# Early expert scores of gathered rows alone, the skip score on VectorE, and values products in the half step of a later unit's scores

## The reference

```python
# 1. attention, B=4, H=8, S=576, D=64; heads 0-3 a local window of 32, heads 4-7 strided by 32
scores = np.where(masks[None], scale * np.matmul(q, k.transpose(0, 1, 3, 2)), -1e9)
attn = softmax(scores)                       # written out with max, exp and sum + 1e-9
x = np.matmul(attn, v)                       # -> (2304, 512)
# 2. dense layer, d_ff = 2048
h = x @ w_in
g = np.where(h >= 1, h, np.where(h <= -1, 0.0, (h + 1) ** 2 / 4))
x = g @ w_out
# 3. experts, E = 8, F = 1024
do_compute = x @ w_skip > 0                  # all other rows are passed on unchanged
xc = x[do_compute]
logits = xc @ w_gate
e_idx = np.argmax(logits, axis=1)            # one expert for each row
gate_w = softmax(logits)[row, e_idx]
out[do_compute] = xc + gate_w * (np.maximum(xc @ w1[e_idx], 0.0) @ w2[e_idx])
```

## Time and profile before

| what | value |
|---|---|
| median of 3 runs | 529.65 us (528.9 to 530.3) |
| the profiled execution's own time | 529.79 us |
| its span, first to last instruction | 527.9 us |
| PE, PEld (weight loads beside PE) | 97%, 83% of the span busy |
| DVE, ACT, POOL | 48%, 39%, 40% |
| granted TensorE clock, mean | 0.983 |

### The profile page before, as it was taken

The page is one execution under the profiler, slowest core; times in us unless marked ns, Lnnn a source line. Parts: engine busy times, 40 slices in busy tenths (PEclk is TensorE's granted clock), DMA queues, the critical chain, the costliest instruction groups (busy, mean ns, idle before and its releaser), DMA issues.

```text
span 527.9 us, 9196 instructions
## 1 busy us (share of the span) xinstructions
PE 512.3 (97%) x3546; PEld 439.2 (83%) x3546; DVE 251.3 (48%) x580; ACT 207.2 (39%) x461; POOL 211.5 (40%) x242
## 2 busy tenths in 40 slices
PE   5899998999999999999999999999999999999996
PEld 3687887889888888888888888888988988887895
DVE  5947657733226435646534646552322483222222
ACT  4956554553332324343433354433232223323122
POOL 0659787662222324544633444542221323221221
PEclk9769999999999999999999999999999999999999
DMA  8992201003001104201210420000300071840001
GB/s 250 343 382 98 70 28 52 31 2 119 1 1 52 64 24 165 76 3 34 91 45 1 166 76 32 2 1 22 115 6 1 0 259 62 299 161 1 2 0 63
DMA packets 19010, 42.22 MB, mean 80 GB/s; under 512 B 2084, under 2 KB 3952, under 8 KB 18964
## 3 DMA queue, kind: packets, MB, share of 16 engines
q1 hardware_dynamic: 18836, 41.59, 22.8%
q0 software_dynamic: 128, 0.02, 0.0%
HBM read 33.06 MB, written 8.78 MB: 79 GB/s over the span
## 4 chain that ended last, share of the span: by engine, by line
PE 88%; DVE 7%; ACT 2%; issue 1%; POOL 1%; DMA 1%; SPq 0%; DVEq 0%; ACTq 0%
PE bank L1004 37%; PE bank L1020 36%; PE bank L865 4%; PE bank L829 4%; PE bank L846 3%; PE bank L875 1%; DVE row_sum L1165 1%; PE bank L886 1%; DVE bank L1148 1%; DVE row_max L1153 1%; DMA qk<-in_qk_dram 1%; DVE prob L1155 1%; PE bank L951 1%; PE bank L932 1%; DVE prob_first L1139 1%
## 5 line engine op out<-in xcount | busy, mean ns | idle before, releaser
L1748 POOL TENSOR_TENSOR g_lo<-act_f,g_hi 128x384 fp32r<-128x384 f32 x96 | 97.1, 1012 | 202.2 <-ACT g_hi L1634 201.9
L1625 ACT ACTIVATE act_f<-act_f,half_col 128x384 f32<-128x384 f32 x96 | 59.2, 616 | 207.4 <-DVE act_f L1367 207.3
L1367 DVE TENSOR_SCALAR act_f<-bank 128x384 f32<-128x384 f32 x96 | 53.2, 554 | 159.7 <-PE bank L1004 155.9
L1004 PE MATMUL bank<-x_hi,win_hi 128*128 128x384 f32 x384 | 90.1, 354 | 0.6 <-DVE act_f L1370 0.6
L1020 PE MATMUL bank<-wout_hi,g_hi 128*128 128x512 f32 x285 | 86.2, 411 | 0.0
L1004 PE MATMUL bank<-x_hi,win_lo 128*128 128x384 f32 x384 | 84.4, 338 | 0.0
L1004 PE MATMUL bank<-x_lo,win_hi 128*128 128x384 f32 x384 | 83.8, 336 | 0.0
L1634 ACT CAST g_hi<-act_f 128x384 fp32r<-128x384 f32 x96 | 49.2, 512 | 84.8 <-DVE act_f L1370 83.9
L1020 PE MATMUL bank<-wout_lo,g_hi 128*128 128x512 f32 x285 | 81.1, 393 | 0.0
L1020 PE MATMUL bank<-wout_hi,g_lo 128*128 128x512 f32 x285 | 80.9, 392 | 0.0
L1004 PEld LDWEIGHTS bank<-x_hi,win_hi 128*128 128x128 f32 x384 | 65.8, 190 | 8.4 <-issue 2.8
(11 more groups left out here) (134 smaller groups left out, 469.2 us busy)
## 6 DMA issues: line engine op xcount, KB each, us to landing
w_early<-in_w_dram SPq DMA_DIRECT2D x4, 2048.0 KB, 8.7
qk<-in_qk_dram SPq DMA_DIRECT2D x12, 592.0 KB, 4.0
out_dram<-y_rows SPq DMA_DIRECT2D x18, 256.0 KB, 2.6
win_raw<-in_w_in_dram SPq DMA_DIRECT2D x16, 256.0 KB, 9.1
wout_raw<-in_w_out_dram SPq DMA_DIRECT2D x16, 256.0 KB, 9.4
y_dram<-y_rows SPq DMA_DIRECT2D x15, 256.0 KB, 2.8
v<-in_v_dram SPq DMA_DIRECT2D x6, 384.0 KB
v<-in_v_dram SPq DMA_DIRECT2D x6, 288.0 KB
```

The source lines that it names most:

```text
L1004: mm = pe.matmul(h_ps[s % 2][:, 0:CH], w[:, f, P * k:P * (k + 1)], x[:, k, cols], start=(at == 0), stop=(at == len(order) - 1))
L1367: dve.tensor_scalar(tile, h_ps[s % 2][:, 0:CH], -1.0, 1.0, ALU.max, ALU.min).then_inc(clip_ready, 1)
L1625: act.activation(tile, tile, ACT.Square, bias=half_col[:, 0:1], scale=0.5).then_inc(square_ready, 1)
L1748: pool.tensor_tensor(g_lo[:, s % RING, :], act_f[:, s % 2, :], g_hi[:, s % RING, :].bitcast(F32), ALU.subtract).then_inc(g_lo_ready, 1)
```

## The change

1. The score jobs `Y`, `Z`, `A` leave the trunk. The skip score of each 128 rows is made on DVE instead (`row_skip`: one 128x512 multiply-and-sum of `y_rows` and `w_skip`, both in SBUF, and its accumulator read), at places 6, 10 and 14 (4, 5, 6 in `c` = 4). The expert scores of all rows are made only in the branch behind the trunk, which now first loads the rows back.
2. The early experts choose rows by the skip score alone (at most 32 rows), from place 7 of `c` = 4 on; the rows are gathered once, turned, and only they are multiplied with `w_gate` (`gate`, 16 calls of 8 columns). Their experts are ranked, the two first experts that are present are loaded, and both tiles work on the same 32 rows; a row is scattered from the tile of its own expert.
3. `w_skip` is loaded at the start of `c` = 1 instead of in `c` = 5.
4. In `c` = 2 and 3 every `V` moves one place back; `S` and `P` stay. In `c` = 1 the second of the two units starts at place 24 instead of 22, and `P` and `V` of both come one place sooner after their `S`.

```diff
     if c == 1:
         for i in range(EARLY, PER_BATCH):
-            unit_at(N_PRO + REST + i, 18 + 4 * (i - EARLY), 5, 7)
+            unit_at(N_PRO + REST + i, 18 + 6 * (i - EARLY), 4, 6)
     if c in (2, 3):
         for i in range(PER_BATCH):
-            unit_at(N_PRO + REST + PER_BATCH * (c - 1) + i, 1 + 3 * i, 4, 5)
+            unit_at(N_PRO + REST + PER_BATCH * (c - 1) + i, 1 + 3 * i, 4, 6)
+    if c > 0:
+        for t, at in enumerate((4, 5, 6) if c == EARLY_CHUNKS else (6, 10, 14)):
+            got[at].append(("skip", CT * (c - 1) + t))
     if c == EARLY_CHUNKS:
-        for i in range(5):
-            got[19 + i].append(("rank", i))
-        got[21].append(("count", 0))
-        got[25].append(("weights", 0))
-        for i in range(2):
-            got[24 + i].append(("choose", i))
-            got[26 + i].append(("info", i))
-            got[27 + i].append(("ids", i))
-            got[28 + i].append(("gather", i))
+        for at, kind in ((7, "flag"), (9, "count"), (11, "slot"), (13, "choose"), (15, "info"), (16, "ids"),
+                         (17, "gather"), (20, "turn"), (22, "gate"), (23, "rank"), (25, "present"), (26, "experts"),
+                         (27, "weights")):
+            got[at].append((kind, 0))
     if c == EARLY_CHUNKS + 1:
-        got[4].append(("skip", 0))
         got[20].append(("left", 0))
...
         for i in range(2):
-            got[i].append(("turn", i))
...
-    if c > 0:
-        for at, job in zip((6, 8, 10, 12, 13, 15, 17), score_jobs(c - 1)):
-            got[at].append(job)
...
-PLACES_AFTER = [score_jobs(CHUNKS - 1)]
+SCORE_ORDER = [CHUNKS - 1] + list(range(CHUNKS - 1))
+PLACES_AFTER = [score_jobs(c) for c in SCORE_ORDER]
...
             for c in range(CHUNKS):
+                if c == 1:
+                    wait_full(sp, "V", N_PRO - 1)
+                    sp.dma_start(w_skip_sb[:, :], w_skip[:, :]).then_inc(w_skip_loaded, 16)
...
+            def early_gates():
+
+                take_bank(pe, "gate", 0)
+                wait_free(pe, "turn", 0)
+                for k in range(KT):
+                    for g in range(4):
+                        mm = pe.matmul(bank_of("gate", 0)[ES * g:ES * (g + 1), 0:E], e_rows_t[:, ES * k:ES * (k + 1)],
+                                       w_score[:, k, 0:E], start=(k == 0), stop=(k == KT - 1))
+                mm.then_inc(full_sem("gate", 0), 1)
...
+            def row_skip(q):
+
+                c, t = q // CT, q % CT
+                if q == 0:
+                    dve.wait_ge(w_skip_loaded, 16)
+                wait_rows(dve, c, t)
+                dve.tensor_tensor_reduce(out=skip_terms[:, :], in0=y_rows[:, t, :], in1=w_skip_sb[:, :], scale=1.0,
+                                         scalar=0.0, op0=ALU.mult, op1=ALU.add, accum_out=score[:, q, E:E + 1])\
+                   .then_inc(row_skips, 1)
+                dve.wait_ge(row_skips, q + 1)
...
                 for t in (0, 2):
                     if c > 0:
                         dve.wait_ge(y_stored[t], 32 * c)
-                        wait_full(dve, "Y", CT * (c - 1) + t)
+                        dve.wait_ge(row_skips, CT * c)
                     dve.tensor_copy(y_rows[:, t, :], y_ps[t][:, :]).then_inc(y_dve, 1)
...
+            def gather_early():
                 pool.wait_ge(e_placed, 4)
...
+                for t in range(CT):
+                    pool.wait_ge(y_stored[t], 32 * EARLY_CHUNKS)
+                pool.wait_ge(e_info_steps, 6)
+                pool.indirect_dma_start(out=e_rows[:, :], out_offset=None, in_=y_quarters[0:4 * P * ET, :],
+                                        in_offset=bass.IndirectOffsetOnAxis(ap=e_row_ids[:, 0:1], axis=0),
+                                        bounds_check=last_quarter, oob_is_err=False).then_inc(e_gathered, 16)
```

More of the change, by code:

```diff
@@ L171, in places_of_chunk @@
             got[8 + 11 * i].append(("second", i))
-    if c > 0:
-        for at, job in zip((6, 8, 10, 12, 13, 15, 17), score_jobs(c - 1)):
-            got[at].append(job)
     return got
 PLACES = [places_of_chunk(c) for c in range(CHUNKS)]
-PLACES_AFTER = [score_jobs(CHUNKS - 1)]
+SCORE_ORDER = [CHUNKS - 1] + list(range(CHUNKS - 1))
+PLACES_AFTER = [score_jobs(c) for c in SCORE_ORDER]
 def bank_table():
     n_banks = {"S": 2, "P": 2, "V": 1, "Y": 1, "Z": 1, "A": 1,
-               "count": 1, "info": 1, "turn": 1, "first": 1, "back": 1, "second": 1, "total": 1}
+               "count": 1, "info": 1, "turn": 1, "gate": 1, "present": 1, "first": 1, "back": 1, "second": 1,
+               "total": 1}
     used = [0] * 8
@@ L765, in _ @@
                             early_weights(n)
-                        if kind == "skip":
-                            sp.wait_ge(h_full, FT * (CHUNKS - 1))
-                            wait_full(sp, "info", 1)
-                            sp.dma_start(w_skip_sb[:, :], w_skip[:, :]).then_inc(w_skip_loaded, 16)
                     if c > 0 and at == 2 * LAG - 1:
@@ new lines, in early_gates, with early_present @@
+            def early_gates():
[6 more added lines that the diff above has]
+                mm.then_inc(full_sem("gate", 0), 1)
+            def early_present():
+                take_bank(pe, "present", 0)
+                pe.wait_ge(e_ranked, 2)
+                pe.matmul(bank_of("present", 0)[:, 0:E], et("ones"), e_onehot[:, :], start=True, stop=True)\
+                  .then_inc(full_sem("present", 0), 1)
@@ L961, in do_jobs @@
                     if kind == "info":
-                        early_info(n)
+                        early_info()
                     if kind == "turn":
-                        turn_early_rows(n)
+                        turn_early_rows()
+                    if kind == "gate":
+                        early_gates()
+                    if kind == "present":
+                        early_present()
                     if kind == "first":
@@ L1182, in keep_scores @@
                 tiles = score_tiles(n)
[L1183 removed]
                 rows = bank_of("A", n)[:, 0:SC * len(tiles)].rearrange("p (t e) -> p t e", e=SC)
[L1185 removed]
+                dve.tensor_copy(score[:, tiles[0]:tiles[-1] + 1, 0:E], rows[:, :, 0:E])\
                    .then_inc(free_sem("A", n), 1)
@@ L1255, in early_choose, with early_flags, early_slots @@
-            def early_choose(i):
+            def early_flags():
+                dve.wait_ge(row_skips, ET)
+                dve.wait_ge(e_table_loaded, 32)
+                early_link(dve.tensor_scalar(e_flags[:, :], score[:, 0:ET, E], 0.0, None, ALU.is_gt))
+            def early_slots():
+                counts = bank_of("count", 0)
+                wait_full(dve, "count", 0)
+                early_link(dve.tensor_tensor_scan(e_running[:, :], et("ones")[:, 0:ET], counts[:, 0:ET], 0.0,
+                                                  ALU.mult, ALU.add))
+                early_link(dve.tensor_scalar(e_over[:, :], e_running[:, ET - 1:ET], float(ES), None, ALU.is_gt))
+                early_link(dve.tensor_tensor(e_slot[:, :], e_running[:, :], counts[:, ET:2 * ET], ALU.subtract))
+                dve.sem_inc(free_sem("count", 0), 1)
+                early_link(dve.tensor_scalar(e_skipped[:, :], e_flags[:, :], 0.0, FAR, ALU.is_equal, ALU.mult))
+                early_link(dve.tensor_tensor(e_slot[:, :], e_slot[:, :], e_skipped[:, :], ALU.add))
@@ L1326, in do_jobs @@
                         count_left()
-                    if kind == "rank":
-                        early_rank(n)
-                    if kind == "choose":
-                        early_choose(n)
-                    if kind == "ids":
-                        early_ids(n)
+                    if kind == "skip":
+                        row_skip(n)
+                    if kind == "flag":
+                        early_flags()
+                    if kind == "slot":
+                        early_slots()
+                    if kind == "choose":
+                        early_choose()
+                    if kind == "ids":
+                        early_row_ids()
+                    if kind == "rank":
+                        early_rank()
+                    if kind == "experts":
+                        early_experts()
                     if kind == "second":
@@ L1420, in first @@
                 dve.wait_ge(r_loaded, 16)
-                for n in range(2 * (CHUNKS - 1), 2 * CHUNKS):
+                for n in range(2 * CHUNKS):
                     wait_free(dve, "A", n)
@@ L1781, in first @@
                 pool.wait_ge(y_kept, 16 * CT)
+                for i in range(2):
+                    pool.wait_ge(e_scattered[i], 16)
                 for i in range(2):
```

335 lines of the change are left out of this document (151 added, 184 removed).

## The result

The changed kernel takes 511.58 us (median of 4 runs, 510.04 to 512.21) against 529.61 us (4 runs, 528.9 to 530.3) for the kernel before: a ratio of 0.9655, 95% interval 0.963 to 0.968, or 18.0 us less. The forecast was 511.0 with a range of 509.3 to 515.5. The profiled execution took 512.21 us, its span is 510.4.

A forecast was written before the change was run, and what follows sets the result against it. PE's work was taken as the bound: 16.4 + 2.5 + 0.3 - 0.5 = 18.7 us off the profiled 529.8 gives 511.1, so 511.0 for the median, range 509.3 to 515.5.

The forecast's parts named there:

- What bounds the kernel: PE, busy 97% of the span, runs without a gap through 96 steps; the time is the sum of its work.
- Score jobs, 16.4 us: Removing five sets of `Y`, `Z`, `A` from the loop, 3.28 us of PE each, saves 16.4 us.
- Shared places, 2.5 us: `V` and `S` sharing a place in `c` = 1, 2 and 3 saves 13 x 0.19 = 2.5 us.
- the transposes' wait, 0.3: In `c` = 1 the 0.27 us wait of `P` behind the next unit's `S` goes, saving 0.3 us.
- `c` = 2 and 3 at 84.1: Sign in the later profile: these chunks take 84.1 us each, 88.53 less a score set and six shares.
- Early experts, 0.5 us: Early path on PE: 34 new short matmuls against 17 gone cost 0.5 us, bounds 0 and 1.4.
- The gather's room: Early chain, places 15 to 20: 9.3 us of work in 10.5 us, 1 us to spare.
- The skips, hidden: 15 `row_skip` on DVE, 0.8 us each, 12 us in all, fit into spare room and cost PE nothing.
- Both are in time by 0.4 to 0.6 us: Places 6 to 8 of `c` = 2: banks of `V` and `S` come free that long before `P` wants them.
- Held skips: Skips blocked by POOL operations make PE wait 0.6 to 1.2 us at four places: 513.5 to 516; chance 0.2.
- rival 1: The prediction's number for Held skips: 2.4 to 4.8 us lost, 513.5 to 516 us; chance 0.2.
- The stopping ring: The bank ring makes PE wait at 13 shared places, 23.1 us with those behind skips: 534.1 us; chance 0.03.

The follow-up runs named there:

- experiment 1: The changed kernel without its moves of `V` and of the `c` = 1 units, so only the score jobs leave; 514.22 us, ratio 0.9707.
- experiment 4: The changed kernel with the matmuls of `Y`, `Z`, `A` put back on PE at their old places, results unused; 533.94 us, ratio 1.0081.
- experiment 2: The kernel before with only the moves of `V` and of the `c` = 1 units, score jobs kept; 530.88 us, ratio 1.0031.
- experiment 6: The changed kernel with 13 of the 15 skips cut to 8 columns; 511.06 us, against 511.42 for the changed kernel run again.
- experiment 7: The changed kernel with the turn of the gathered rows at place 18 of `c` = 4 instead of 20; 513.22 us, ratio 0.969.
- experiment 5: The changed kernel with each of its 15 skips done three times, 522.52 us, and in a second kernel twice, 517.34 us.
- experiment 3: The changed kernel with score banks in `c` = 2 and 3 freed only after mask, maximum and subtraction, the subtraction on DVE; 527.11 us, ratio 0.9963.

## Why the prediction was right

**What bounds the kernel.** Right: PE's work, without gaps. Every experiment that gave PE work or a wait in the loop lengthened the chunk by about that. ("The others of the loop are under 1 us each" passes over one wait of 1.0 us for ACT in `c` = 0, which all kernels have.)

**Score jobs, 16.4 us.** Measured 15.0: experiment 1 gives it with the early path in it, which cost nothing (below). Putting the products back gave 15.5 (experiment 4, waits taken off), there in a table in which fewer of them stand beside a `V`. The mis-sized step is "A set costs 3.28 us. Five sets lie in the loop": `c` = 1, 4 and 5 have 3.24, 2.98 and 3.40, but `c` = 2 and 3 only 2.70, where the jobs stand in places that already hold small products. I had priced the merging of small products for the shares and not for these.

**Shared places, 2.5 us, and the transposes' wait, 0.3.** 3.1 for both. The price of a share was right: 0.18 us in experiment 1 against 0.19. What the sum lacks is the last two `V` of `c` = 2 and 3, which share nothing: 0.4 us a chunk, mostly a wait for POOL that went, less the 0.24 that `c` = 3 lost at place 17. The sum also treats the gain as standing alone, but it needs the other part of the change: in the kernel before the moves cost 1.1 us (experiment 2). It came out right only because both parts were made.

**The total.** 18.7 was forecast and 18.1 measured in the loop. That this is so close is partly luck: the score jobs gave 1.4 less than priced, the early path cost 0.5 less and the moves gave 0.3 more.

**`c` = 2 and 3 at 84.1.** 84.35 and 84.59. The 0.24 between them is the `P` of place 17 in `c` = 3, which the narrow skips bring back (experiment 6).

**Early experts, 0.5 us.** This part was not run by itself. By `c` = 4 and 5: two sets by experiment 4 are 3.14 + 3.21 = 6.35, the chunks lost 2.98 + 3.39 = 6.37. So the early path costs PE about nothing, at the lower bound. The gate's 32 short products are cheaper than the row I took them from, 0.4 us in all instead of 1.0 (a product's own time is 179 ns where the earlier trace rows has 274, and the 32 start within 0.3 us); in the kernel after the group is

```profile
L931 PE MATMUL bank<-w_score,e_rows_t 128*32 128x8 f32 x32 | 0.4, 179 | 0.0
```

The gather's room was 1.9 us, not 1, and experiment 7 shows what it is worth.

**The skips, hidden.** Right but for the 0.24 us at place 17 of `c` = 3, a place that the prediction did not work out. The one that it did, places 6 to 8 of `c` = 2, in the kernel after:

```profile
208.08 0.55 DVE L1409 TENSOR_TENSOR act_f<-act_f,bank 128x384 f32<-128x384 f32 x1
...
209.81 0.71 DVE L1195 TENSOR_TENSOR x_lo<-bank,x_hi 128x288 fp32r<-128x288 f32 x1 [1.18 <-ACT x_hi L1570]
...
210.84 0.82 DVE L1159 SCALAR_TENSOR_TENSOR prob<-bank,mask_s 72x288 f32<-72x288 f32 x2 [0.31 <-DVE x_lo L1195]
211.27 0.66 PE L844 MATMUL bank<-ident,prob 72*72 72x72 f32 x8
```

`x_lo` ends at 210.53, 0.7 us before `P` starts at 211.27. A mask takes 0.45 us, so the first of the two frees `S`'s first bank at 211.29, and the second half of `P` starts at 211.52, its first weights at 211.46. "Both are in time by 0.4 to 0.6 us" was too little for `V`'s bank and too much for `S`'s: there it is 0.2, since the mask starts 0.31 us behind `x_lo`, a wait that I had left out. The places with such a `P` are also six (8, 14 and 17 in `c` = 2 and 3), not the four that I had counted. A hold like that of experiment 5's second skip, 0.35 us, would have shown.

**Held skips.** Given a chance of 0.2, and close, as the room was 0.2 us. The Trainium skill (SBUF — State Buffer, "Who interferes with whom") says that of two such instructions the later one is blocked fully. The traces agree on how much the loser loses: a whole skip or a POOL operation that loses ends 0.52 to 0.69 us behind the other's end, having done most or all of its work after it. Six of the 15 skips of the kernel after met a POOL pair, and none was held (0.64 to 0.68 us each); POOL was. At place 6 that fits the order too, since the skip of 207.40 began 0.16 us before POOL, as the prediction had argued. At place 10 it does not: POOL began 0.20 us before the skip and lost. So rival 1 stayed away by the prediction's argument at place 6, and by luck at place 10. Held were a second skip straight behind the first, which began while a POOL operation stood (1.03 to 1.54 us), and the narrow skip of place 10 (0.49 instead of 0.11). What decides between two that begin so close was not settled.

**The stopping ring.** Rightly given little, by the right reason: with the late release it costs 1.35 us a place (experiment 3), and in experiment 2 the ring did stop PE, where a score job stood behind `V` and `S` in one place.

## What to carry to other kernels

Where one engine is busy without a gap, price a change by what that engine is spared at the place where the work stood: here a small product beside another small one was cheaper than the same alone between long ones. Moves that only merge such products were worth about 0.2 us each here, and only while the next user of the bank ring came late enough: write down, for each place, which bank the next user takes and which operation frees it. "Hidden" is a number of its own; double the added operation once, and the room that is left can be read from the chunk's length.

## What was unexpected of the hardware

A multiply-and-sum on DVE over two SBUF inputs of 128x512 took 0.68 to 0.69 us alone and 0.64 to 0.68 where a POOL pair also read SBUF, while the pair went from 1.29 to 1.63 and 2.03 us. The second one, straight behind the first (0.03 us after its accumulator read), took 1.03, 1.19 or 1.54 us where POOL was at work and 0.69 where it was not. POOL's record began 0.20 us ahead of the skip at place 10 in both kernels of experiment 6: with 512 columns POOL was the one held, with 8 columns the skip. And leaving the program took 3.4 us longer in one kernel (experiment 4), where SP waited 3.6 instead of 0.2 us for PE's sequencer after the last result was written.
